# Another written-out order of work inside each head pair of a fused attention and expert kernel

## The reference

```python
q_pool = q.reshape(B, H, S // 2, 2, D).mean(axis=3)      # B 4, H 8, S 1152, D 64
attn = softmax(q_pool @ k^T / sqrt(D))                   # 576 x 1152 for each head
x = (attn @ v) laid out as 2304 rows x 512
x = moe(x)        # 8 experts, top 1, 512 -> 1024 -> 512
out = swiglu(x)   # 512 -> 1536 -> 512
```

## Time and profile before

| | us |
|---|---|
| median of 3 runs | 1480.11 (1476.28 to 1482.66) |
| the profiled execution, its own time | 1476.28 |
| its span, first to last instruction | 1474.5 |
| first issue of body 1 to that of body 14 (78.89 to 540.03) | 461.14 |
| attention, about | 0 to 607 |

### The profile page before, as it was taken

The page is one execution under the profiler, slowest core; times in us unless marked ns, Lnnn a source line. Parts: engine busy times, 40 slices in busy tenths (PEclk is TensorE's granted clock), DMA queues, the critical chain, the costliest instruction groups (busy, mean ns, idle before and its releaser), DMA issues. The chain is left out here.

```text
span 1474.5 us, 24891 instructions
## 1 busy us (share of the span) xinstructions
PE 1377.8 (93%) x7733; PEld 1195.3 (81%) x7734; DVE 873.2 (59%) x1658; ACT 638.4 (43%) x1549; POOL 345.2 (23%) x241
## 2 busy tenths in 40 slices
PE   3999999999999999739978999998999999999998
PEld 2788888888888888537767787887999999999997
DVE  2899999999999998673443444445632323223232
ACT  2888888788888887532034102004411111111111
POOL 3122222222222220279179205022101010100000
PEclk9999999999999999969998999999999999999999
DMA  7566666666666764356256313114400000000000
GB/s 164 124 139 139 138 138 142 146 144 145 145 149 145 195 132 153 101 193 247 88 199 233 116 43 107 43 57 142 150 32 15 29 15 17 26 0 21 0 22 22
DMA packets 127931, 156.85 MB, mean 106 GB/s; under 512 B 47633, under 2 KB 86545, under 8 KB 125841
## 3 DMA queue, kind: packets, MB, share of 16 engines
q1 hardware_dynamic: 111968, 114.35, 30.8%
q10 hardware_dynamic: 12880, 31.99, 6.5%
q0 software_dynamic: 3040, 9.96, 2.0%
HBM read 87.33 MB, written 29.10 MB: 79 GB/s over the span
## 5 line engine op out<-in xcount | busy, mean ns | idle before, releaser
L514 ACT ACTIVATE p_hi<-ps_t 128x512 fp32r<-128x512 f32 (+1 forms) x336 | 194.3, 586 | 69.1 <-PE ps_t L694 64.7
L657 DVE TENSOR_TENSOR p_lo<-ps_t,p_hi 128x512 fp32r<-128x512 f32 (+1 forms) x336 | 216.9, 666 | 12.4 <-ACT p_hi L514 7.8
L578 DVE TENSOR_REDUCE maxima<-ps_s 128x1 f32<-128x512 f32 x288 | 193.7, 686 | 41.5 <-PE ps_s L792 37.7
L538 ACT ACTIVATE probs<-ps_s,neg_max 128x512 f32<-128x512 f32 x288 | 198.6, 690 | 44.1 <-DVE neg_max L591 43.9
L792 PE MATMUL ps_s<-kq_t 128*128 128x512 f32 x640 | 199.7, 414 | 13.6 <-DMA kq_t<-kept_rows 9.5
L694 PE MATMUL ps_t<-ident,probs 128*128 128x128 f32 x1296 | 198.5, 274 | 1.4 <-DVE kept_rows L569 0.8
L1026 POOL TENSOR_TENSOR w_parts<-raw_w,w_parts 128x1024 fp32r<-128x1024 f32 x64 | 150.9, 2396 | 184.5 <-ACT w_parts L1096 184.4
L694 PEld LDWEIGHTS ps_t<-ident,probs 128*128 128x128 f32 x1296 | 156.0, 140 | 46.3 <-DVE p_lo L657 9.6
L1642 ACT ACTIVATE silu<-ps_g 128x384 f32<-128x384 f32 x72 | 35.4, 491 | 314.6 <-PE ps_g L1748 314.6
L1695 DVE TENSOR_TENSOR silu<-ps_g,silu 128x384 f32<-128x384 f32 x72 | 40.1, 558 | 210.7 <-ACT silu L1642 210.7
L1096 ACT ACTIVATE w_parts<-raw_w 128x1024 fp32r<-128x1024 f32 x64 | 67.1, 1059 | 220.0 <-PE ps_h L1423 104.2
(11 more groups left out here) (190 smaller groups left out, 2786.5 us busy)
## 6 DMA issues: line engine op xcount, KB each, us to landing
raw_w<-in_moe_w ACTq DMA_DIRECT2D x61, 512.0 KB, 4.1
kq_t<-kept_rows SPq DMA_DIRECT2D x32, 608.0 KB, 6.2
kq_t<-kept_rows SPq DMA_DIRECT2D x32, 320.0 KB, 7.1
raw_k<-in_k SPq DMA_DIRECT2D x32, 288.0 KB, 5.7
raw_v<-in_v SPq DMA_DIRECT2D x16, 576.0 KB, 5.5
kq_t<-kept_rows SPq DMA_DIRECT2D x32, 288.0 KB, 6.5
raw_q<-in_q SPq DMA_DIRECT2D x32, 256.0 KB, 4.1
y_by_slot<-x_out SPq DMA_DIRECT2D x25, 256.0 KB, 2.0
```

The lines of the kernel that those rows point to most:

```text
L514: nc.scalar.activation(p_hi[prob_ring(kind, m)][:, 0:w], T[ring(kind, j)][:, 0:w], ACT.Copy).then_inc(hi_ready, 1)
L538: nc.scalar.activation(probs[:, at:at + 512], S[(2 * tile + h) % SR][:, :], ACT.Exp, bias=neg_max[:, tile:tile + 1], accum_out=sums[par][: ...
L578: nc.vector.reduce_max(maxima[:, 3 * tile + h:3 * tile + h + 1], S[(2 * tile + h) % SR][:, :], AX).then_inc(max_done, 1)
L657: nc.vector.tensor_tensor(p_lo[n][:, 0:w], t[:, 0:w], p_hi[n][:, 0:w].bitcast(F32), ALU.subtract).then_inc(t_free, 1)
```

## The change

Only four lists differ. The computation is the same and so is every instruction's form; their order on PE, ACT and DVE differs. ("g", 0) is moved from tenth place to the first of the list. The other g steps move by one or two places, some a, c and x steps change places with them, and scores, maxima and exponentials are put behind other steps.

```diff
     UNITS = [
-        ("b", 0), ("b", 1), ("b", 2), ("b", 3), ("b", 4), ("b", 5), ("b", 6), ("b", 7), ("b", 8),
-        ("g", 0), ("g", 1), ("c", 0), ("c", 1), ("c", 2), ("g", 2), ("a", 0), ("g", 3), ("a", 1),
-        ("a", 2), ("x", 0), ("a", 3), ("x", 1), ("a", 4), ("a", 5), ("a", 6), ("a", 7), ("a", 8),
+        ("g", 0), ("b", 0), ("b", 1), ("b", 2), ("b", 3), ("b", 4), ("b", 5), ("b", 6), ("b", 7),
+        ("b", 8), ("g", 1), ("c", 0), ("c", 1), ("g", 2), ("c", 2), ("g", 3), ("a", 0), ("a", 1),
+        ("x", 0), ("x", 1), ("a", 2), ("a", 3), ("a", 4), ("a", 5), ("a", 6), ("a", 7), ("a", 8),
     ]
-    SCORES_AT = [(26, 26), (2, 2), (4, 5), (7, 8), (12, 13), (17, 17), (19, 20), (21, 22), (23, 24)]
-    MAXIMA_AT = [(25, 25), (2, 2), (3, 4), (7, 8), (12, 13), (16, 16), (18, 19), (20, 21), (22, 23)]
-    EXP_AT = [(0, 2, 2), (4, 4, 4), (7, 8, 8), (11, 11, 13), (16, 16, 17), (18, 19, 20), (21, 21, 21), (22, 23, 23), (25, 25, 25)]
+    SCORES_AT = [(25, 26), (2, 3), (5, 6), (8, 9), (12, 13), (14, 16), (18, 18), (21, 22), (24, 24)]
+    MAXIMA_AT = [(25, 26), (2, 2), (4, 6), (8, 9), (11, 12), (14, 15), (17, 18), (20, 21), (22, 23)]
+    EXP_AT = [(2, 3, 3), (5, 6, 6), (8, 9, 9), (11, 12, 13), (14, 15, 15), (18, 19, 19), (20, 21, 22), (22, 23, 24), (25, 25, 26)]
```

## The result

The changed kernel takes 1609.44 us (median of 4 runs, 1605.13 to 1610.95) against 1481.18 before (4 runs): a ratio of 1.0867, interval 1.0833 to 1.0902. The forecast was 1617, on the profiled execution; that one took 1604.07 us, with a span of 1602.3. Ratios are of fast runs alone, which leaves out one run of the experiments (3223.4 us, of the kernel before with v first).

What follows compares the result with a forecast made beforehand. PE and DVE together bound the kernel before. After the change, body 0's issue at 53.3, fourteen L (299.3), 14 x 0.14 and 13 x 23.3 give 657.5 against 519.2; with body 14's 2.5, +141 on 1476.3: 1617 us, range 1580 to 1636.

Steps and rivals of the forecast that it cites:

- What bounds before: Body of the kernel before: PE and DVE together, busy 35.07 and 32.85 of 35.45 us, no engine waiting for a transfer.
- 4.96 us to spare: Kernel before: ("g", 0) of the next body starts on PE 4.96 us behind the end of L, which stays hidden.
- L: Transfer chain from SP's first copy issue through the k and q loads to POOL's last sum: 21.4 us on average.
- The stall: PE at ("g", 0), now first in the body, waits 6.2 us for the end of L, unfilled.
- L unchanged: The transfer chain does not shrink: same transfers, same queue; fourteen of them sum to 299.3 us.
- T = 23.3: From start of ("g", 0) to SP's next issue: 21.0 us plus 2.3 us for PE's low clock after the wait.
- The half us on T: ("g", 0) to SP's next issue at full clock: before's 20.83 us plus 0.2, 21.0, DVE's work nearly the same.
- Body 0: Exponentials of tiles 0 to 2 now stand behind ("g", 0): SP's first issue at 53.3 us against 44.34.
- Rival A: PE's clock stays up after the wait, T is 21.0: 1585 us; chance 0.12.
- Rival B: Restart costs more: low clock lasts about 6.8 us, 1632 us, or maxima and exponentials add waits to T; chance 0.10.
- Rival C: Transfers come in time, L 15.3 us or less, no stall; new order saves 14 us, 1462; chance 0.02.
- Rival D: PE has other work ahead of the wait, or ("g", 0) is late anyway: 1476 to 1480 us; chance 0.02.

Runs made afterwards that it cites:

- v first: Load of v put ahead of the loads of k and q on SP's queue, against the kernel before: 1481.03 us, ratio 1.0.
- stall filled: Changed kernel with 60 extra transposes of the identity on PE ahead of the wait of g0 in the mid bodies: 1579.31 us.
- the new tail: Kernel before, keeping its first ten steps and entries for tiles 1 to 3 (exponentials 0 to 2), everything behind from the changed kernel: 1477.71 us, ratio 0.9965.
- the small loads: Changed kernel whose six loads of k and q move one row of 64 numbers each for pairs 2 to 15: 1524.15 us.
- behind b2: Kernel before with ("g", 0) moved to stand behind ("b", 2), three of nine b steps ahead of it: 1546.92 us, ratio 1.0438.

## Why the prediction was right, point by point

- *What bounds before, and 4.96 us to spare.* Right, except that POOL did wait for a transfer (its sums for the load of q, 86.0 us in 200 to 500), which held nobody up. Adding 2.2 us to L was free in the old order and cost a full 2.15 us a body in the new one.
- *The stall.* Right in place and releaser. I gave it 6.2 us; it was 6.6 to 6.8 in most bodies and 7.3 to 8.3 in the first three. The 0.7 us that I let the last g step move ahead did not come: PE was there 14.52 us after the issue, and not 15.3. The stall's length was not in the sum.
- *L unchanged.* Right: 298.9 us for the fourteen against 299.3.
- *T = 23.3.* The mechanism was right and the size too large. The fourteen T sum to 315.0, 22.5 each, against 23.3 + 0.14. Both terms were over: at the full clock T is 20.5 (stall filled), against 21.0 + 0.14, and the clock costs 2.0, not 2.3. These 0.94 us a body, 13 us in all, are about the distance between 1617 and the profiled 1604. The low clock lasted 4.6 us on average behind the release (half-microsecond windows over the fourteen bodies), which is what I had taken; but it cost 0.43 of that time, not half.
- *The half us on T.* Here two errors offset each other, which was luck. I took DVE's work in T as the same as in before's 20.83 us. It is 18.03 us (3.77 + 14.26 with the stall filled) against 19.74, 37 instructions against 41. I had read the operation at 236.40 as DVE's first b step: the first of its two is the last a step of the body before, whose fill ACT had copied at 234.71, and in front of it, from 235.40 on, DVE still finished maxima of that body. The changed kernel does such leftovers in the stall. Against these 1.7 us less of work, DVE idles 2.4 us in T instead of 1.1, the start without stock (1.46 us until its first operation at 245.32) among them, which I had let cancel. The balance is the 0.4 us by which T is shorter than 20.83.
- *Body 0.* 53.3 forecast, 52.69 measured, and for the reason given: ACT does the exponentials of tiles 0 to 2 behind g0, at 38.32, 41.32 and 44.33, 3.0 us apart.
- *Rival A (clock stays up, 1585).* It was not what happened, but the filled stall makes it happen, at 1579.
- *Rival B.* The low clock lasted up to 6.1 us in single bodies, beyond the 5.7 seen before, but even there T was 23.05, below 23.44. The maximum of tile 4 a step ahead of its scores, which I named as a danger, did no net harm: the new tail, which contains it, is a little faster.
- *Rival C (transfers in time, 1462).* L never came near 15.3. Its price was too hopeful as well: without the stall the new tail is worth 0.35%, about 5 us, and not 14, and the rest of the order as a whole costs 0.4%.
- *Rival D.* Excluded by the wait that is there.

## What to carry to other kernels

When a step is moved in a hand-written order, look up what it waits for and what it releases, and add up the loop through both: here the g steps release the transfers that the next g0 waits for, and a body can be no shorter than the chain of transfers plus the work from the first g step to the last. A transfer that is hidden has a margin that one can read (4.96 us here), and a move within it is nearly free: past it every us counts once a body, and there is more to pay where PE's wait lets its clock fall. A lag counted in places rather than in named steps makes a harmless-looking shift of a list into a wait between two engines.

## What the hardware showed beyond that

- Sixty useless transposes in front of a wait made the kernel 30 us faster, as they kept PE at 2.4 GHz: T fell from 22.5 to 20.5.
- Behind waits of 2.4 to 3.5 us the clock fell in some bodies and not in others of the same kernel (in five of fourteen with the small loads), and not by the wait's length: behind b2 it stayed up after 3.49 us and fell with 2.63. In four bodies of that kernel it fell only 0.9 to 1.2 us after PE had resumed. Behind the waits of 6.3 us and more in bodies 1 to 14 it fell in each.
- What a fall costs varies with how long the clock stays low once PE works again. In this body (window of the changed kernel, from the release at 339.05) it was low for the 2.80 us shown and T was 21.8, whereas the body above, low for 5.5 us, had 22.8, and the longest, low for 6.1 us, 23.05.

```profile
339.05:341.85 2.80, 2.80 (x11) 2.50 (x12) 0.69 (x1) 0.60 (x1) 0.00 (x0) 0.50 0.47 170
```

- Making transfers tiny does not remove their place in the queue: six loads of 64 numbers left L at 17.0 of 21.3 us. SP was busy issuing for 13.5 of these, 204.93 to 218.43: the copies first, then 3.94 us for the six. How much of that is the cost of an issue and how much full DMA engines, no run separates.
